# Attention and two feed-forward layers on one core: the probabilities become the stationary operand of the mix, and x is turned after it is divided

## The reference

```python
scores = q @ k.T / sqrt(64) - slope[h] * dist      # kept: first n_global = 8 keys, n_local = 96 keys back
a = exp(scores - max); a = a / (sum(a) + 1e-9)
x = (a @ v), heads side by side                    # 1536 x 512
h = x @ w_in; solu = h * softmax(h)                # 1536 x 1024
y = layernorm(solu) * g_ln @ w_out                 # 1536 x 512
yn = y / rms(y) * rms_g
out = (silu(yn @ w_gate) * (yn @ w_val)) @ w_down  # inner width 1536
```

## Time and profile before

| | |
|---|---|
| median of 3 runs | 591.17 us (591.16 to 591.57) |
| profiled execution, its own time | 591.57 us |
| its span | 589.8 us |
| PE busy | 558.5 us, 95% of the span |
| DVE, ACT, POOL busy | 52%, 45%, 16% |

### The profile page before, as it was taken

The page is one execution under the profiler, slowest core; times in us unless marked ns, Lnnn a source line. Parts: engine busy times, 40 slices in busy tenths (PEclk is TensorE's granted clock), DMA queues, the critical chain, the costliest instruction groups (busy, mean ns, idle before and its releaser), DMA issues.

```text
span 589.8 us, 10771 instructions
## 1 busy us (share of the span) xinstructions
PE 558.5 (95%) x3697; PEld 480.2 (81%) x3697; DVE 307.1 (52%) x790; ACT 265.5 (45%) x610; POOL 93.9 (16%) x223
## 2 busy tenths in 40 slices
PE   2786999999999999999999999999999999999997
PEld 1564777777777777768899999999999999999996
DVE  4769878877887898767465132222212222222221
ACT  3668666776677786746443212222221222222112
POOL 4541122124202223323000010000001000000000
PEclk9997999999999999999999999999999999999999
DMA  8656662444244422414340200020020000001000
GB/s 216 193 148 183 198 174 77 125 125 125 76 125 125 127 76 76 159 57 176 111 170 9 73 1 1 1 72 0 1 72 0 0 0 36 0 0 37 1 1 36
DMA packets 21613, 46.95 MB, mean 80 GB/s; under 512 B 2764, under 2 KB 2776, under 8 KB 21576
## 3 DMA queue, kind: packets, MB, share of 16 engines
q1 hardware_dynamic: 21264, 46.47, 26.2%
q10 hardware_dynamic: 312, 0.01, 0.0%
HBM read 40.18 MB, written 6.29 MB: 79 GB/s over the span
## 4 chain that ended last, share of the span: by engine, by line
PE 80%; DVE 10%; POOL 4%; issue 3%; ACT 1%; DMA 1%; ACTq 0%; DVEq 0%; SPq 0%
PE hidden L413 9%; PE hidden L414 8%; PE hidden L415 8%; PE mixed L1265 3%; PE turned L413 3%; PE turned L414 3%; PE mixed L413 3%; PE scores_a L413 3%; PE mixed L414 3%; PE scores_b L413 3%; PE scores_a L414 3%; PE scores_b L414 3%; PE scores_b L415 3%; PE scores_a L415 3%; PE turned L415 3%
## 5 line engine op out<-in xcount | busy, mean ns | idle before, releaser
L741 ACT ACTIVATE act_hi<-act_sb 128x256 fp32r<-128x256 f32 x72 | 30.2, 420 | 108.8 <-DVE act_sb L1121 108.8
L1121 DVE TENSOR_TENSOR act_sb<-mixed,silu 128x256 f32<-128x256 f32 x36 | 15.3, 425 | 94.1 <-PE mixed L415 93.9
L1121 DVE TENSOR_TENSOR act_sb<-turned,silu 128x256 f32<-128x256 f32 x36 | 15.3, 424 | 88.6 <-PE turned L415 85.9
L413 PE MATMUL hidden<-down_hi,act_hi 128*128 128x512 f32 x144 | 56.9, 395 | 0.1
L414 PE MATMUL hidden<-down_lo,act_hi 128*128 128x512 f32 x144 | 56.9, 395 | 0.0
L415 PE MATMUL hidden<-down_hi,act_lo 128*128 128x512 f32 x144 | 56.7, 394 | 0.0
L685 ACT ACTIVATE probs_t<-turned 116x512 f32<-116x512 f32 x48 | 28.7, 598 | 54.9 <-PE turned L1250 54.9
L1126 DVE TENSOR_TENSOR act_lo<-act_sb,act_hi 128x256 fp32r<-128x256 f32 x72 | 30.6, 426 | 35.0 <-ACT act_hi L741 35.0
L675 ACT ACTIVATE probs<-logits,neg_max 128x232 f32<-128x232 f32 x96 | 45.8, 481 | 6.0 <-DVE neg_max L1008 6.0
L413 PE MATMUL hidden<-in_hi,xt_hi 128*128 128x512 f32 x96 | 42.8, 446 | 0.9 <-DVE xt_lo L1031 0.5
L413 PE MATMUL turned<-yt_hi,val_hi 128*128 128x256 f32 x144 | 40.8, 283 | 0.0
(11 more groups left out here) (147 smaller groups left out, 1540.2 us busy)
## 6 DMA issues: line engine op xcount, KB each, us to landing
qk_raw<-qk_pairs SPq DMA_DIRECT2D x96, 180.0 KB, 3.2
v_in<-v_windows SPq DMA_DIRECT2D x12, 448.0 KB
staging<-w_gate SPq DMA_DIRECT2D x3, 1024.0 KB, 7.4
staging<-w_val SPq DMA_DIRECT2D x3, 1024.0 KB, 5.8
y_spill<-y_out SPq DMA_DIRECT2D x12, 256.0 KB, 3.9
staging<-w_down SPq DMA_DIRECT2D x3, 1024.0 KB, 5.9
y_in<-y_spill SPq DMA_DIRECT2D x6, 512.0 KB, 3.9
out<-o_sb SPq DMA_DIRECT2D x12, 256.0 KB, 2.1
```

Source lines behind the costliest of these rows:

```text
L413: pe.matmul(acc, hi, other_hi, start=first, stop=False)
L741: nc.scalar.activation(act_hi[:, slot], act_sb[:, slot], ACT.Copy).then_inc(act_rounded, 1)
L1121: nc.vector.tensor_tensor(act_sb[:, slot], val_ps[slot][:, 0:WIDE], silu[:, slot], ALU.mult).then_inc(act_ready, 1)
```

## The change

The mix has its operands exchanged: the turned probabilities are stationary (116 x 128), v streams (64 columns), and each head gives a 128 x 64 block of x with positions on the partitions. Two products of a head now follow each other before the next head comes. The reciprocals no longer have to be turned: `turn_recip`, `copy_recip` and the spreading copy go, and `normalise_x` makes the reciprocal itself at p = 0 and multiplies with it broadcast. Instead x itself is transposed on PE after the division (`turn_x`, 4 transposes, after `turn_pair` at p = 0; in the first pass at the very front of p = 0, ahead of `score_pair`). ACT rounds it from PSUM and DVE subtracts from PSUM. PE, no longer ACT, waits for `x_final`. On DVE, `apply_norm` at p = 1 moves from behind `split_qk` to in front of it. The general path is changed in the same way; these inputs do not take it.

```diff
             def round_x(t, even):
-                act.wait_ge(x_final, 16 * (t + 1))
+                act.wait_ge(xt_ready, t + 1)
...
-                nc.scalar.activation(xt_hi[:, even], x[:], ACT.Copy).then_inc(xt_rounded, 1)
+                nc.scalar.activation(xt_hi[:, even], turned_x[:], ACT.Copy).then_inc(xt_rounded, 1)
...
-            def invert_sums(a, even):
+            def normalise_x(a, even):
                 dve.wait_ge(probs_ready, heads * (a + 1))
                 nc.vector.tensor_scalar(denom[:], exp_sum[:, even], 1e-9, None, ALU.add).then_inc(denom_steps, 1)
...
                 nc.vector.reciprocal(recip[:], denom[:]).then_inc(denom_steps, 1)
...
+                dve.wait_ge(mixed_ready, pairs * (a + 1))
                 if not known(a) or a >= 1:
-                    dve.wait_ge(recip_turned, a)
-                nc.vector.tensor_copy(recip_wide[:], recip[:].unsqueeze(2).to_broadcast([P, heads, d])
-                                      ).then_inc(denom_steps, 1)
-
-            def normalise_x(a):
-                dve.wait_ge(recip_copied, a + 1)
-                dve.wait_ge(mixed_ready, pairs * (a + 1))
-                nc.vector.tensor_tensor(x[:], mixed[:].rearrange("p (c n) -> p c n", c=pairs), x[:],
+                    dve.wait_ge(xt_ready, a)
+                nc.vector.tensor_tensor(x[:], mixed[:].rearrange("p (h d) -> p h d", h=heads),
+                                        recip[:].unsqueeze(2).to_broadcast([P, heads, d]),
                                         ALU.mult).then_inc(x_ready, 1)
...
+                    if p == 1 and is_tile(t - 1):
+                        apply_norm(t - 1)
                     if p == 2 and is_tile(t - 1):
                         split_ln(t - 1, 0)
...
                     split_qk(n + 2, (p + 2) % pairs)
-                    if p == 1 and is_tile(t - 1):
-                        apply_norm(t - 1)
...
-                for half in range(2):
-                    for h in range(2):
-                        head = 2 * p + h
-                        ins = pe.matmul(mixed[h * d:(h + 1) * d, p * P:(p + 1) * P],
-                                        v_in[:, even, half, head * d:(head + 1) * d], probs_t[:, p % 2, h, half],
+                for h in range(2):
+                    head = 2 * p + h
+                    for half in range(2):
+                        ins = pe.matmul(mixed[:, head * d:(head + 1) * d], probs_t[:, p % 2, h, half],
+                                        v_in[:, even, half, head * d:(head + 1) * d],
                                         start=(half == 0), stop=(half == 1))
...
+            def turn_x(t):
+                pe.wait_ge(x_final, 16 * (t + 1))
...
+                for k in range(KM):
+                    ins = pe.transpose(turned_x[:, k * P:(k + 1) * P],
+                                       x[:].rearrange("p h d -> p (h d)")[:, k * P:(k + 1) * P], ident[:])
+                ins.then_inc(xt_ready, 1)
...
                     first = known(t) and t == 0
+                    if first and p == 0:
+                        turn_x(t)
                     score_pair(n + 1, (p + 1) % pairs)
...
                     turn_pair(n, p)
-                    if p == 3 and is_tile(a):
-                        turn_recip(a)
+                    if p == 0 and not first:
+                        turn_x(t)
```

More of the change, by code:

```diff
@@ L62, in fused_kernel @@
     assert 2 * d == P and model == BANK and N1 == 2 and K1 == N1 * KJ and KM == KJ and HALF * 2 == WIN
-    x_general = nc.dram_tensor("x_general", (tiles, P, pairs * P), F32, kind="Internal").ap()
+    x_general = nc.dram_tensor("x_general", (tiles, P, model), F32, kind="Internal").ap()
     y_dram = nc.dram_tensor("y_spill", (tiles, P, model), F32, kind="Internal").ap()
@@ L152, in fused_kernel @@
             assert at <= SPARE
-            x = sbuf(one, "x", [P, pairs, P])
-            recip_wide = sbuf(one, "recip_wide", [P, heads, d])
+            x = sbuf(one, "x", [P, heads, d])
             xt_hi = sbuf(one, "xt_hi", [P, 2, KM, P], F32R)
@@ L252, in fused_kernel @@
         gen_x_ready = sem("gen_x_ready")
+        xt_ready = sem("xt_ready")
         xt_rounded = sem("xt_rounded")
@@ L1030, in split_x @@
                 dve.wait_ge(xt_rounded, t + 1)
-                nc.vector.tensor_tensor(xt_lo[:, even], x[:], xt_hi[:, even].bitcast(F32), ALU.subtract
-                                        ).then_inc(xt_split, 1)
+                nc.vector.tensor_tensor(xt_lo[:, even], turned_x[:].rearrange("p (k n) -> p k n", k=KM),
+                                        xt_hi[:, even].bitcast(F32), ALU.subtract).then_inc(xt_split, 1)
             def max_hidden(t, n):
@@ L1133, in one_tile @@
                     if p == 0 and is_tile(t):
-                        normalise_x(t)
+                        normalise_x(t, even)
                     if p == 3 and is_tile(t):
@@ L1261, in mix_pair @@
                     pe.wait_ge(x_ready, a)
-                for half in range(2):
-                    for h in range(2):
-                        head = 2 * p + h
-                        ins = pe.matmul(mixed[h * d:(h + 1) * d, p * P:(p + 1) * P],
-                                        v_in[:, even, half, head * d:(head + 1) * d], probs_t[:, p % 2, h, half],
+                for h in range(2):
[3 more added lines that the diff above has]
+                                        v_in[:, even, half, head * d:(head + 1) * d],
                                         start=(half == 0), stop=(half == 1))
                 ins.then_inc(mixed_ready, 1)
[L1270 to L1276, removed]
+            def turn_x(t):
+                pe.wait_ge(x_final, 16 * (t + 1))
+                if not known(t) or t >= 2:
+                    pe.wait_ge(ln_split, N1 * (t - 1))
+                elif t == 1:
+                    pe.wait_ge(xt_split, 1)
                 else:
                     pe.wait_ge(cols_ready, 1)
[L1279 to L1282, removed]
+                for k in range(KM):
+                    ins = pe.transpose(turned_x[:, k * P:(k + 1) * P],
+                                       x[:].rearrange("p h d -> p (h d)")[:, k * P:(k + 1) * P], ident[:])
+                ins.then_inc(xt_ready, 1)
             def ffn_in(t, even, n, ks):
@@ L1330, in turn_y @@
                         pe.wait_ge(ln_split, N1 * (tiles - 1))
-                        pe.wait_ge(recip_copied, tiles)
+                        pe.wait_ge(xt_split, tiles)
                     elif known(b) and b == 1:
@@ L1436, in attend_tile @@
                     for j in range(seq):
-                        ins = pe.matmul(mixed[0:d, 0:P], gen["v"][:, j * d:(j + 1) * d],
-                                        gen["probs_t"][:, j * P:(j + 1) * P], start=(j == 0), stop=(j == seq - 1))
+                        ins = pe.matmul(mixed[:, 0:d], gen["probs_t"][:, j * P:(j + 1) * P],
+                                        gen["v"][:, j * d:(j + 1) * d], start=(j == 0), stop=(j == seq - 1))
                     ins.then_inc(gen_mixed, 1)
```

28 lines of the change are left out of this document (10 added, 18 removed).

## The result

The changed kernel takes 595.54 us (median of 6 runs, 594.61 to 596.37), the kernel before 591.45 in the same comparison (6 runs, 591.16 to 591.68). The ratio is 1.0068, 95% interval 1.0055 to 1.0082: slower by 4.1 us. Its profiled execution took 596.7 us with a span of 594.9, that is 5.1 more than the profiled execution of before. The forecast was 593.1, 1.9 slower: the direction came as forecast, the loss is twice that.

A forecast was written before the change was run, and what follows sets the result against it. PE, busy 95% of the span, was taken as the bound. First tile +1.9, steady tiles +0.3 and last tile -0.3 gave +1.9 on the profiled 591.57: 593.5, or 593.1 as median; range 589.4 to 598.

The forecast's parts named there:

- The mix on PE: Each pair's mix on PE becomes bound by eight loads of 128 columns at 0.11 us: +0.08 a pair, +0.33 a tile.
- Rival (a): In the mix, plain fp32 loads are as fast as a transpose's: 0.29 us less a pair, 590 in all; chance 0.22.
- Turning x: Four transposes of x on PE cost 0.44 us like the four old ones, with no wait in a steady tile.
- the 0.31: Per tile on PE, the wait of 0.26 us before the old transposes and 0.05 of exposed load go.
- The sum's 19.65: PE's period per tile if PE alone set it: 19.63 - 0.31 + 0.33 us.
- The chain through DVE and POOL: From one p = 2 score group to the next, it just meets PE: period 19.65 to 19.75, +0.3 us in all.
- The first tile: turn_x ahead of the scores on PE delays the first input product to 35.2: +1.9 us, bounds 0 and +2.4.
- The end: At the last tile PE waits less before x: about -0.3 us.
- Rival (b): POOL does not get its 0.89 back; PE idles 0.45 to 0.9 us a tile before p = 2 scores: 597 to 601; chance 0.17.
- Rival (c): The first tile's delay costs nothing, since PE has waits after it, and the rest stands: 591.3 us; chance 0.16.

The follow-up runs named there:

- e5: e3 with 128 columns of v streamed per head in the mix instead of 64 (x is then not the reference's): 591.5 us, ratio 1.0001.
- e7: e3 with 96 of the 128 stationary columns of the probabilities in the mix, from the second tile on: 588.15 us, ratio 0.994.
- e3: The changed kernel with apply_norm back behind split_qk and the first tile's turn_x behind score_pair: 591.82 us, ratio 1.0006.
- e6: The kernel before with turn_recip on PE just ahead of the mix at p = 3 and copy_recip behind exp_pair on ACT: 591.63 us, ratio 1.0001.
- e1: The changed kernel with only apply_norm put back behind split_qk at p = 1: 593.52 us, ratio 1.0025.
- e8: e6 with the copy that spreads the reciprocals moved from DVE to ACT, behind exp_hidden at p = 3: 588.89 us, ratio 0.9956.
- e4: The kernel before with apply_norm alone moved ahead of split_qk at p = 1: 600.3 us, ratio 1.0147.
- e9: e8 with ACT's spreading copy behind the exponentials in the first tile alone: 587.52 us, ratio 0.994.
- e2: The changed kernel with only the first tile's turn_x put behind score_pair on PE: 594.31 us, ratio 1.0047.

## Why the prediction was right on the direction and short on the size

**The mix on PE.** Right. 1.22 was worked out from the last product to the second score record; it is 1.23, so +0.10 a pair for +0.08. Rival (a) is out: a record takes 0.101, and e5 and e7 show the load as the cause. By the formula of the Trainium skill, "TensorE: Matmul & The Clock Gate", section "LDWEIGHTS (loading the stationary operand)", a load takes an estimated 107 ns for 128 columns and 80 for 96. At full pace the traces come near (101 and 78). The Trainium skill, "TensorEngine Tiling (Array Packing)", section "When to Use Tiling", counsels half-array tiles at 64 columns. Here they gained no time: e3 is level with the half-array form.

**Turning x.** Right: four transposes in 0.44, no wait in a steady tile. But the 0.31 that the sum credits to the wait alone is not to be had alone: e6 takes away the same wait in the kernel before and the period stays, because a second loop, through DVE, was level with PE. The sum's 19.65 came out all the same (19.66 in e1 and e3). That is luck in part: the change also takes the spreading copy off DVE, and e8 shows that the two together are worth 0.42. Four times the 0.10 of the mix on top of e8's 19.16 and 19.37 gives 19.56 and 19.77, 0.1 under e3; this last step is worked out, not measured.

**The chain through DVE and POOL.** The mechanism was right, the size off, and this is the first term that was mis-sized: +0.3 for the ten periods, and +2.5 measured. POOL was worked out at 4.20 and takes 4.18 in a steady tile; `xt_lo` in its PSUM form does not hold it. The Trainium skill, "SBUF — State Buffer", section "SBUF: two separate sides", lets a DVE operation shut out a GpSimd operation that reads SBUF when it has two SBUF inputs. The step of 0.19 beside `xt_lo`, which has one, agrees, and so does the 1.29 beside `gate_lo`, which has two. What I left out are that one tile, which the trace of before could have shown (a step of 1.25 at 218.08), and two hand-overs. The multiplication for x starts 0.20 after the end of the reciprocal just ahead of it (119.09 to 119.28); I had x at 11.17 after the period's start and it is at 11.34. That is so in all six tiles of the real loop, as the timeline of DVE shows at the last of them and the first behind it:

```profile
179.10 0.20 DVE L1003 RECIPROCAL recip<-denom 128x8 f32<-128x8 f32 x1
179.50 0.69 DVE L1008 TENSOR_TENSOR x<-mixed,recip 128x512 f32<-128x512 f32 x1 [0.20 <-DVE recip L1003]
...
199.04 0.20 DVE L1003 RECIPROCAL recip<-denom 128x8 f32<-128x8 f32 x1
199.28 0.69 DVE L1008 TENSOR_TENSOR x<-mixed,recip 128x512 f32<-128x512 f32 x1
```

In the six tiles written out the gap is 0.04. The instruction has three waits, and in the loop their values depend on the turn; that this is the 0.16 was not tried. And the score stands 0.13 behind the end of `split_qk` (127.73 to 127.86), not 0.05. This too is so in the loop: in e4, where PE stands waiting for it, it is 0.13 to 0.14 in the loop and 0.05 to 0.06 behind it. The period behind the loop, 19.67 (188.07 to 207.74) for 19.51, is longer by 0.16, where those in the loop are longer by 0.3 to 0.4. With the two hand-overs the chain is 19.92 and not 19.69, while PE was due at 19.66 (e1's period). I wrote that the two "meet" and the move adds no more than a tenth. When two loops are level, every error in the longer one goes straight into the period: about 0.25 a tile between this kernel and e1, and 1.2 in the tile with the step of 1.29. That the steady tiles alone lose 2.5 would be a wrong reading of e1: they give a little over half of it. Why every second period is 0.2 longer (20.15) stays open.

**The first tile.** The second mis-sized term: +1.9 was predicted, +3.2 came. The steps are nearly right (x at 30.80 as worked out, the product at 34.95 for 35.2). What failed is the sentence that took the delay of the first product for the whole: another 1.55 came behind it. From the first product to the group it is 9.51 before and 11.07 after. All profiles together sort this out: where PE's products are at full pace by 39.6 us the distance is 9.5 (before, e4 to e9), where they are not before 42.9 it is 10.7 to 11.2 (the changed kernel twice, e1 to e3). e3, e5 and e7 have the same order, and their first products start at 34.10, 34.11 and 34.09; e3's full pace came at 43.5, that of e5 and e7 at 38.3 and 38.7. So the 1.5 us go with the later pace in all twelve profiles, and the order does not fix it. Of the kernels that transpose x five profiles had it late and two early, of the others all five early. The two early ones are those whose mix differs (e5 streams more, e7 loads less), and they ran on another chip; what decides it stays open. The times of e1 fall into two groups, 591.8 to 592.1 (4 runs) and 593.1 to 594.3 (7), 1.8 us apart on average, and those of the changed kernel into 594.6 to 595.1 (3) and 595.9 to 596.4 (3), with the profiled 596.7 beside the upper ones. The size fits an early and a late pace, but the start can be read in the profiled run alone, so this is argued.

In the window view the granted clock stands at 1.00 for 38 to 44 us in both kernels, although the products of the changed one are 0.43 apart there; e5 is the one trace whose clock is recorded earlier, and it shows the lower level:

```profile
34.00:38.00 4.00, 3.89 (x12) 3.31 (x13) 1.12 (x3) 4.00 (x9) 1.53 (x1) 0.50 1.05 286
```

There its products stand 0.43 apart too (34.70, 35.13). At the lower level (1.2 GHz) the whole group of the mix costs more as well: in the changed kernel it takes 1.56 to the score (37.68 to 39.24), 0.195 a record.

**The end, and the rivals.** The stretch of the last tile gave 0.7 back for the 0.3 expected. The wait that shrank there is not the one before x but that of `turn_ln` for `gated`: 0.98 before (259.47) and 0.20 after (264.41). Rival (b) came in part. In a steady tile the score at p = 2 is late by 0.24 instead of 0.45 to 0.9, and by the hand-overs, not by POOL; in one tile it is rival (b) as written, with POOL's chain at 5.10 and a wait of 0.58 on `qk_hi`. e4 shows the full price of the order, +9. Rival (c) is out: e2's group is 1.1 earlier and its time 1.2 lower, e3's group is 0.75 earlier than e1's and its profiled execution 0.8 shorter, so the start is passed on.

## What to carry to other kernels

Moving a step in front of another on an engine that is idle a sixth of the time costs nothing only while its chain is clearly shorter than the period; work out all loops of the pipeline, each from its own hand-overs, and if two are within 0.1 us take the larger error as the change. And look at every tile, not only at a steady one: a step that another engine holds up in one tile cost as much here as five steady tiles. An engine's wait is worth what the next loop leaves of it: removing PE's wait gave 0, removing 0.43 us of DVE's work on top gave 0.4 a tile, though PE was 95% busy. Making the wide operand the stationary one trades streaming for loading, and with few columns streamed the load is the price.

## What the runs showed of the chip that I had not expected

- A load of fp32 weights follows the granted clock here: 0.101 us a record of the mix at full pace, 0.195 at half (1.56 / 8). The load-bound mix is thus dearest at the start, where a pair takes 0.51 more than the half-array form (37.62 to 38.67 in e8: 1.05).
- The same pair of instructions on DVE has 0.04 us between them where the tiles are written out and 0.20 in the real loop; from DVE's `split_qk` to PE's score it is 0.05 and 0.13.
- In e4 the granted clock is 0.50 for 3 us right behind a wait of PE of 1.69 us, in the middle of stage 1.
- The same spreading copy takes 0.43 us on DVE and 0.63 on ACT, and the kernel is faster with the slower one.
